# Two units of an inverse transform moved between stages of the next half, and the loads and products for that half made earlier, in a long-convolution and MLP kernel

## The reference, cut to what matters

```python
h_filt = (np.maximum(pos_emb @ w1, 0.0) @ w2) * window        # 12480 x 128
u = x * v
Uf = np.fft.rfft(u, n=2 * S, axis=1)                          # S = 12480
Hf = np.fft.rfft(h_filt, n=2 * S, axis=0)
y = np.fft.irfft(Uf * Hf[None, :, :], n=2 * S, axis=1)[:, :S, :]
x = x * y                                                      # then 12480 tokens of 128
x = np.maximum(x @ moe_w_in, 0.0) ** 2 @ moe_w_out             # 128 -> 2048 -> 128
h = x @ moe2_w_in
out = h * (1 / (1 + np.exp(-1.702 * h))) @ moe2_w_out
```

## Time and profile before

| what | value |
|---|---|
| timed runs | 1421.34 us median; 1411.77, 1421.34, 1422.18 |
| profiled execution | 1423.75 us, of which the span 1421.9 us |
| TensorE busy | 1411.5 us (99%), mean granted clock 0.993 |
| first half: stages 1, 2, 3, 4 begin at | 20.3, 65.6, 136.9, 165.7 us |
| second half: stages 1, 2, 3, 4 begin at | 202.65, 229.1, 276.85, 305.6 us |
| first MLP matmul | 323.5 us |

### The profile page before, as it was taken

The page is one execution under the profiler, slowest core; times in us unless marked ns, Lnnn a source line. Parts: engine busy times, 40 slices in busy tenths (PEclk is TensorE's granted clock), DMA queues, the critical chain, the costliest instruction groups (busy, mean ns, idle before and its releaser), DMA issues.

```text
span 1421.9 us, 22644 instructions
## 1 busy us (share of the span) xinstructions
PE 1411.5 (99%) x8370; PEld 1398.4 (98%) x8370; DVE 851.5 (60%) x1092; ACT 1000.6 (70%) x1422; POOL 190.2 (13%) x157
## 2 busy tenths in 40 slices
PE   9999999999999999999999999999999999999999
PEld 9999999999999999999999999999999999999998
DVE  6745416745666666666666666666666666666664
ACT  7654325555877777777777777777777777777776
POOL 5545533551000000000000000000000000000000
PEclk9999979999999999999999999999999999999999
DMA  8254352642000000000000000000000000000000
GB/s 250 67 160 125 81 143 70 187 139 76 0 19 19 18 18 18 18 18 18 18 18 18 18 18 18 18 18 18 18 18 18 18 18 18 18 18 18 6 7 12
DMA packets 32646, 63.75 MB, mean 45 GB/s; under 512 B 3964, under 2 KB 24876, under 8 KB 32348
## 3 DMA queue, kind: packets, MB, share of 16 engines
q1 hardware_dynamic: 32064, 62.76, 15.4%
q10 hardware_dynamic: 540, 0.42, 0.1%
HBM read 50.38 MB, written 6.39 MB: 40 GB/s over the span
## 4 chain that ended last, share of the span: by engine, by line
PE 96%; DMA 2%; ACT 1%; DVE 1%; issue 0%; POOL 0%; POOLq 0%; ACTq 0%
PE ps L1106 25%; PE ps L1108 25%; PE ps L1107 25%; PE ps L792 5%; PE ps L802 4%; PE ps L423 3%; PE ps L849 3%; PE ps L855 3%; PE ps L827 1%; DMA f_ring<-in_inv 1%; ACT big L596 1%; DMA f_ring<-in_fwd 0%; POOL big L380 0%; PE ps L773 0%; PE ps L808 0%
## 5 line engine op out<-in xcount | busy, mean ns | idle before, releaser
L1094 DVE TENSOR_TENSOR act_lo<-act_f,act_hi 128x832 fp32r<-128x832 f32 x480 | 487.9, 1027 | 120.9 <-ACT act_hi L1050 112.7
L1106 PE MATMUL ps<-act_hi,w_hi 128*128 128x416 f32 x960 | 338.4, 353 | 0.7 <-DVE act_lo L1094 0.7
L1106 PE MATMUL ps<-in_hi,w_hi 128*128 128x416 f32 x960 | 336.6, 351 | 0.0
L1107 PE MATMUL ps<-act_lo,w_hi 128*128 128x416 f32 x960 | 336.2, 350 | 0.0
L1108 PE MATMUL ps<-act_hi,w_lo 128*128 128x416 f32 x960 | 336.0, 350 | 0.0
L1108 PE MATMUL ps<-in_hi,w_lo 128*128 128x416 f32 x960 | 335.6, 350 | 0.0
L1107 PE MATMUL ps<-in_lo,w_hi 128*128 128x416 f32 x960 | 335.0, 349 | 0.0
L1092 DVE CAST act_hi<-act_f 128x832 fp32r<-128x832 f32 x240 | 142.6, 594 | 291.8 <-ACT act_f L1045 291.8
L1040 ACT ACTIVATE relu<-ps 128x832 f32<-128x832 f32 x240 | 208.1, 867 | 130.7 <-PE ps L1108 126.6
L1047 ACT ACTIVATE act_f<-ps 128x832 f32<-128x832 f32 x240 | 207.4, 864 | 102.1 <-PE ps L1108 102.1
L1045 ACT ACTIVATE act_f<-relu 128x832 f32<-128x832 f32 x240 | 216.1, 900 | 21.8
(11 more groups left out here) (74 smaller groups left out, 1089.5 us busy)
## 6 DMA issues: line engine op xcount, KB each, us to landing
f_ring<-in_fwd SPq DMA_DIRECT2D x52, 240.0 KB, 2.7
big<-in_inv SPq DMA_DIRECT2D x26, 338.0 KB
big<-in_x_by_channel SPq DMA_DIRECT2D x16, 390.0 KB
big<-in_v_by_channel SPq DMA_DIRECT2D x16, 390.0 KB
x_tile<-in_x_by_tile SPq DMA_DIRECT2D x30, 208.0 KB, 2.7
xy_tile<-big SPq DMA_DIRECT2D x60, 104.0 KB, 2.5
out<-yT SPq DMA_DIRECT2D x30, 208.0 KB, 1.9
big<-in_pos_by_pair SPq DMA_DIRECT2D x15, 208.0 KB, 5.3
```

What stands on the lines that cost most here:

```text
L1094: nc.vector.tensor_tensor(lo[:, :, :], f[:, :, :], hi[:, :, :].bitcast(F32), ALU.subtract)\
L1106: nc.tensor.matmul(to, w_hi[w][:, cols], hi, start=first, stop=False)
L1107: nc.tensor.matmul(to, w_hi[w][:, cols], lo, start=False, stop=False)
```

## The change

- Units 13 and 14 (`KEPT`) of the first half's stage 4 are done in the second half: unit 13 in PSUM slot 1 between stages 1 and 2, unit 14 in slot 2 between stages 2 and 3. Their rows of `Y`, their tables and the last table stay in SBUF till then; for that `h_spec`, `by_re` and `by_im` have other places in the second half.
- The tables have 12 places in the first half; tables 12, 13 and 14 go to the places of 0, 2 and 3 (`T4_AGAIN`). Tables 2, 3 and the last lie over the staging of x and v.
- x and v of pieces 0 to 4 are loaded at two different steps of stage 2; pieces 5 to 7 in stage 3, piece 7 in piece 6's place. GpSimd makes pieces 0 to 3 between its additions of stage 2, and doesn't wait for the stage's end before piece 4.
- The raw weights 0 and 1 are loaded after the second half's stage 2, between tables.
- The last group of stage 2 is split into 8 and 56 channels (before: 32 and 32), and TensorE waits for the second part at step 2 of stage 3 (before: 8).
- The last group of stage 3 is split: VectorE does the first 12 rows of `Y` first and signals `y_first`; stage 4 waits for that and for three of the four slots.
- Spare products: none before the second half's stages 2 and 3, three of one each at the other stage ends.

```diff
 XV_AT = (...,
-         [XV_TOP - (PIECES_AHEAD - i) * XV for i in (*range(PIECES_AHEAD), 4, 3, 4)])
+         [XV_TOP - (PIECES_AHEAD - i) * XV for i in (*range(PIECES_AHEAD), 3, 4, 4)])
+BY_AT = SPEC_AT + 2 * 3 * FG * HC, P1_END
+KEPT_T4_AT = P1_END + 2 * 2 * 2 * FG * HC
+H_SPEC_AT = SPEC_AT, IM_AT
+KEPT = JG - 2, JG - 1
+S4_UNITS = JG - len(KEPT), JG - LATE
+KEPT_SLOT = 1, 2
...
-    t4_places = [[(ring_rows, n * TB * TAB) for n in range(2)]
+    t4_places = [[(ring_rows, n * TB * TAB) for n in range(2)] + [(big, KEPT_T4_AT + n * TB * TAB) for n in range(2)]
                  + [(big, X_AT[0] + X_SIZE + n * TB * TAB) for n in range(8)],
...
+    T4_AGAIN = {T4S[0]: 0, T4S[0] + 1: 2, T4S[0] + 2: 3}
...
-    PARTS = [slice(0, HC // 2), slice(HC // 2, HC)]
+    PARTS = [slice(0, PC), slice(PC, HC)]
+    FIRST_ROWS = (RING - 1) * TB
...
-    def y_made(eng, h):
+    def y_begun(eng, h):
 
-        for q in range(RING):
+        for q in range(RING - 1):
             eng.wait_ge(free[q], used["s3 end", h][q])
+        eng.wait_ge(y_first, h + 1)
...
         for k in range(RING, NG):
             load_f(0, k)
-            if k % RING == RING - 1:
-                load_u(1, k // RING - 1)
+            if k % 2 and k // RING <= PIECES_AHEAD:
+                load_u(1, k // RING - 1, (k % RING // 2,))
 
         p_made(sp, 0)
         stage_done(sp, "s2", 0)
         for g in range(2):
             load_t4(sp, 0, g)
+        for i, consumed in ((5, 3), (6, 4), (7, 6)):
+            sp.wait_ge(u_folded, PIECES + consumed + 1)
+            load_u(1, i)
+        sp.dma_start(w2bd, out_net[:, 2 + D:]).then_inc(w2_in, 16)
+        sp.wait_ge(u_folded, 2 * PIECES)
+        for g in range(2, 4):
+            load_t4(sp, 0, g)
         sp.dma_start(t4_last[0], inv4[:, JG * TB * TAB:]).then_inc(t4_last_in, 16)
-        sp.dma_start(w2bd, out_net[:, 2 + D:]).then_inc(w2_in, 16)
 
         stage_done(sp, "s3", 0)
-        for g in range(2, T4S[0]):
+        for g in range(4, T4S[0]):
             load_t4(sp, 0, g)
-        sp.wait_ge(u_folded, PIECES + 4 + 1)
-        load_u(1, 5)
         load_t4_behind(0, range(T4S[0], JG))
-        sp.wait_ge(u_folded, PIECES + 3 + 1)
-        load_u(1, 6)
-        sp.wait_ge(u_folded, PIECES + 5 + 1)
-        load_u(1, 7)
 
         stage_done(sp, "s4", 0)
         for k in range(NG):
             load_f(1, k)
-        for m in range(2):
-            load_w(m)
-
         p_made(sp, 1)
+        sp.wait_ge(p_rest, 2)
+        load_w(0)
         stage_done(sp, "s2", 1)
-        for g in range(T4S[1]):
+        for g in range(2):
+            load_t4(sp, 1, g)
+        sp.wait_ge(full[KEPT_SLOT[1]], used["kept", 1] + 1)
+        load_w(1)
+        for g in range(2, T4S[1]):
             load_t4(sp, 1, g)
...
                 combine_p(nc.gpsimd.tensor_tensor, k, h, k % 2)
+                i, step = k // RING - 2, k % RING
+                if h == 0 and 0 <= i < PIECES_AHEAD - 1:
+                    if step == 0:
+                        multiply(1, i)
+                    elif step < 3:
+                        fold(1, i, step - 1)
             if h == 0:
 
-                p_made(pool, 0)
-                stage_done(pool, "s2", 0)
-                for i in range(PIECES):
+                for i in range(PIECES_AHEAD - 1, PIECES):
                     make_u(1, i)
...
+        def keep_kept(unit):
+
+            q = KEPT_SLOT[unit]
+            act.wait_ge(full[q], used["kept", unit] + 1)
+            keep_xy(nc.scalar.copy, 0, KEPT[unit], q).then_inc(free[q], 1)
...
             step1_odd(k, h, *act_copies(k, h)).then_inc(last_odd, 1)
+            if h == 1:
+                keep_kept(0)
...
             copy_last_h()
+            if h == 1:
+                keep_kept(1)
             act.wait_ge(p_rest, h + 1)
...
                 dve.wait_ge(im_copied, h * N3 + k + 1)
+                if k == N3 - 1:
+                    rows = slice(0, FIRST_ROWS)
+                    nc.vector.tensor_tensor(low[:, :, rows], re2[:, :, rows], im2[:, :, rows], ALU.subtract)
+                    nc.vector.tensor_tensor(high[:, :, rows], re2[:, :, rows], im2[:, :, rows], ALU.add).then_inc(y_first, 1)
+                    low, high, re2, im2 = (rows[:, :, FIRST_ROWS:] for rows in (low, high, re2, im2))
...
+        def step4_kept(unit):
+
+            q = KEPT_SLOT[unit]
+            pe.wait_ge(free[q], used["kept", unit])
+            step4(pe, 0, KEPT[unit], q, full[q])
...
+            else:
+                step4_kept(0)
             for s in range(RING):
-                if h == 0 and s % 2 == 0:
+                if h == 0 and s % 2 == 0 or h == 1 and s == KEPT_SLOT[0]:
                     continue
                 pe.wait_ge(free[s], used["s1 end", h][s])
-                if h == 1 and s < RING - 1:
-                    spare_products(s, 1)
...
-            for k, spare in ((NG - 4, 2), (NG - 3, 1), (NG - 2, 2)):
-                q, n = product_slot(k, 1)
-                if h == 0:
-                    q, n = hidden_slot(k)
-                    before, m = product_slot(k - 1, 0)
-                    pe.wait_ge(free[before], m + 1)
+            if h == 1:
+                step4_kept(1)
+            for k in (NG - 4, NG - 3, NG - 2) if h == 0 else ():
+                q, n = hidden_slot(k)
+                before, m = product_slot(k - 1, 0)
+                pe.wait_ge(free[before], m + 1)
                 pe.wait_ge(free[q], n + 1)
-                spare_products(q, spare)
+                spare_products(q, 1)
             p_made(pe, h)
 
             for k in range(N3):
-                if k == N3 // 2:
+                if k == PC // 4:
                     pe.wait_ge(p_rest, h + 1)
                 step3(k, h)
 
-            for k, spare in ((N3 - 4, 1), (N3 - 3, 2), (N3 - 2, 2)):
+            for k, spare in ((N3 - 4, 1), (N3 - 3, 1), (N3 - 2, 1)):
...
-            y_made(pe, h)
-            for g in range(JG - h * LATE):
+            y_begun(pe, h)
+            for g in range(S4_UNITS[h]):
```

More of the change, by code:

```diff
@@ L273, in convolution, with t4_slot @@
     T4S = [len(slots) for slots in t4]
-    T4_USES = [len(range(n, JG, T4S[0])) for n in range(T4S[0])]
-    t4_last = [ring_rows[:, 2 * TB * TAB:2 * TB * TAB + TAB], big[0:A, T4_AT[1] + 5 * TB * TAB:W_LO2_AT]]
+    T4_AGAIN = {T4S[0]: 0, T4S[0] + 1: 2, T4S[0] + 2: 3}
+    T4_USES = [1 + (n in T4_AGAIN.values()) for n in range(T4S[0])]
+    t4_last = [big[0:A, at:at + TAB] for at in (KEPT_T4_AT + 2 * TB * TAB, T4_AT[1] + 5 * TB * TAB)]
+    def t4_slot(h, g):
+        if h:
+            return g % T4S[1], T4_USES[g % T4S[1]] + g // T4S[1] + 1
+        return (T4_AGAIN[g], 2) if g in T4_AGAIN else (g, 1)
     def x_and_v(h, i):
@@ L312, in convolution @@
     last_copied, part_negated = sem("last_copied"), sems("part_negated", 2)
-    part_made, p_rest = sem("part_made"), sem("p_rest")
+    part_made, p_rest, y_first = sem("part_made"), sem("p_rest"), sem("y_first")
     p_done = sems("p_done", 2)
@@ L318, in convolution @@
     for h in range(2):
-        for name, groups in (("s1", N1[h]), ("s2", (2 - h) * NG), ("s3", N3), ("s4", JG - h * LATE)):
+        for name, groups in (("s1", N1[h]), ("s2", (2 - h) * NG), ("s3", N3), ("s4", S4_UNITS[h])):
             used[name, h] = list(n)
@@ L322, in convolution @@
             used[name + " end", h] = list(n)
+            if h == 1 and name in ("s1", "s2"):
+                unit = ("s1", "s2").index(name)
+                used["kept", unit] = n[KEPT_SLOT[unit]]
+                n[KEPT_SLOT[unit]] += 1
     F_USES = [len(range(s, NG, RING)) for s in range(RING)]
@@ L373, in product_slot @@
         return q, used["s2", h][q] + (k // RING if h else k // 2)
-    PARTS = [slice(0, HC // 2), slice(HC // 2, HC)]
+    PARTS = [slice(0, PC), slice(PC, HC)]
+    FIRST_ROWS = (RING - 1) * TB
     def combine_p(tensor_tensor, k, h, half):
         to = P[h][:, :, :, k * FG:(k + 1) * FG].rearrange("p c r f -> p r c f")
-        tensor_tensor(to, by_re[:, half], by_im[:, half], ALU.add).then_inc(p_done[half], 1)
+        tensor_tensor(to, by_re[h][:, half], by_im[h][:, half], ALU.add).then_inc(p_done[half], 1)
     def after(eng, sem, n):
@@ L412, in step4 @@
     def step4(pe, h, g, q, done):
[L414 to L415 removed]
+        n, loads = t4_slot(h, g)
+        pe.wait_ge(t4_in[n], 16 * loads)
         blocks = [(0, i, t4[h][n][:, i]) for i in range(TB)]
@@ L462, in load_pe, with load_u @@
                 .then_inc(ld_pe[n], 16)
-        def load_u(h, i):
+        def load_u(h, i, both=(0, 1)):
             c = h * HC + i * PC
-            for to, rows in zip(x_and_v(h, i), (x_ch, v_ch)):
-                sp.dma_start(to, rows[:, c:c + PC, :]).then_inc(ld_u[i], 16)
+            for n in both:
+                sp.dma_start(x_and_v(h, i)[n], (x_ch, v_ch)[n][:, c:c + PC, :]).then_inc(ld_u[i], 16)
         def load_f(h, k):
@@ L545, in _, with multiply, fold, make_u @@
     def _(pool):
-        def make_u(h, i):
+        def multiply(h, i):
```

(22 more changed lines are left out.)

18 lines of the change are left out of this document (9 added, 9 removed).

## The result

The changed kernel takes 1429.9 us (six runs, 1428.6 to 1430.8). Before takes 1413.4 (six runs, 1411.4 to 1422.2, with the three known ones among them). The ratio is 1.0104, with a 95% interval of 1.0077 to 1.0131: slower by 1.0%, where I forecast 1405. Two things are in that number. The changed kernel loses 23 us in one place (its profile shows the place; its six runs lie within 2.2 us of each other), and before doesn't usually lose the 10 us of clock that I took out of it: over all series 17 of its 64 runs lie at 1421 or more, the others between 1411 and 1415.

The account below looks back on a forecast made before the run. TensorE, busy 99% of the span, was taken to bound the kernel. From the profiled execution, 1423.75-12.0-0.3-3.65-1.6+0.5+0.15=1406.8, a usual run 2 under: 1405 us; range 1401 to 1419.

Parts of the forecast that it names:

- The tables' queue: SyncE's loads for the first half's stage four: table 2 lands 0.5 us before its need; 0.5 us of later waits.
- the rival: First half's stage four: table 2 late, TensorE idles 1.5 us at unit 2, clock falls; 1424 us, chance 0.12.
- 12.0 us on one transfer: First half's stage four in before: a late table costs 2.0 us idle plus the clock's fall; all 12.0 go.
- The price of the fall: Lower clock in before: 7.5 us in stage four's last 84 records, 2.5 us in the second half's stage one.
- The units: Units 13 and 14 moved from the first half's stage four into the second half's gaps: net -3.65 us.
- First rows: End of stage three: first rows done apart start stage four 0.8 us earlier in both halves, -1.6 us.
- U made in stage two: First half: GpSimd's pieces 0 to 3 fit between its combines of stage two, cost zero.
- The 0.3 us for the forward table: Loading x and v at different steps may remove a 0.4 us table wait; 0.3 us gain taken.
- Weights 0 and 1 later: Second half: loading them between tables from about 278.5 costs zero, with ScalarE up to 2 us late.
- First channels: Start of stage three: 8 and 56 channels gain nothing, cost zero up to 0.5; 0.15 us added.
- Spare products: Stage-end gaps: fewer of them cost no time, since other engines end those gaps.
- rival b: Start of stage three: VectorE's first add loses to GpSimd's product, TensorE idles some 3 us; 1450 us, chance 0.06.

Follow-up runs that it names:

- experiment 1: Changed kernel with table places swapped: tables 2 to 9 where P was, 10, 11 and the last over the staging of x and v; 1406.4 us.
- experiment 2: Changed kernel with pieces 5 and 6 of x and v issued ahead of tables 0 and 1 in the first half's stage three; 1406.7 us.
- experiment 5: The kernel before, unchanged, run for a second profile; 1412.2 us (one run).
- experiment 4: The kernel before with piece 5 of x and v issued behind tables 10 to 13 instead of ahead of table 10; 1412.6 us, ratio 0.9972.
- experiment 12: Kernel of 8 with the first rows apart undone and five spare products (1, 2, 2) before the first half's stage four; 1406.7 us.
- 8: Kernel of experiment 1 with the first half's last two stage-four units in order 12, 11 and table 12 issued ahead of 11; 1405.6 us.
- experiment 10: Kernel of 8 with the first channels apart undone (32 and 32, second part wanted at step 8); 1405.7 us.
- experiment 9: Kernel of 8 with the first rows apart undone, three spare products kept before stage four; 1406.6 us in one run, 1427.8 to 1427.9 in three.
- experiment 6: Changed kernel with three spare products in front of unit 2 of the first half's stage four; six runs 1408.0 to 1410.0, four 1427.9 to 1430.9 us.
- experiment 3: Changed kernel with eight spare products in front of unit 2 of the first half's stage four, table 2 still late; 1409.2 us.

## Why the prediction was wrong

**The step that failed** is in "The tables' queue": "Table 2 lands at 168.0", with a margin of 0.5 us. Stage three began at 135.95 instead of 136.9, so in this trace's times I had piece 5 at 144.4, the last fold at 163.9, table 2 at 167.1 and the need at 167.6. Measured: piece 5 at 146.15 (+1.7), piece 7 5.9 us after its issue (+0.6), table 2 3.7 us after its own (+0.5). That is 2.8 us late against 0.5 of margin. GpSimd's 4.7 us per piece, the need and the order of events were right. The term that was too small is the landing time of a piece. It came from one median landing of a 240 KB load plus bytes over a mean rate, and three such prices stand one behind the other in a chain in which each piece waits for the one before.

Three things show what was missing. First, experiments 1 and 2 show that the chain decides: with table 2 outside it, or with piece 5 issued first, the wait is gone. Second, a piece with nothing ahead of it takes 5.9 to 6.4 us (piece 7 in the profile after, pieces 5 and 7 in experiment 2), not 5.3. Third, piece 5 didn't have the queue to itself behind the two tables: some 0.6 MB of piece 6 went over before it had landed, and my sum stopped at piece 5's own bytes. How much of the 1.7 us this last part makes is open; no run holds piece 6 back. The prediction had a row that would have warned it: it worked out 1.86 us per table for before, where other loads stood behind too, and used that for the tables from number 2 on, but the faster 209 GB/s (1.66 us per table) for the pieces. At 1.86 us per 338 KB piece 5 would have landed 9.4 us after the issue, piece 7 after 5.7, and table 2 would have been late by 0.8 us.

**The second error is of weighing.** The prediction had the rival and its mechanism, at 1424 us and a chance of 0.12, and I took the margin as if it were safe. I gave the chance that GpSimd is 1 us late too little, and the range ended at 1419. Its size was off by 6 us: the wait was 2.4 and not 1.5, the fall cost 18.0 in the units and not 15.6, 2.9 and not 2.5 in stage one, and the kernel without it takes 1406.4 and not 1405. The price of the units was low because the factor 1.79 was taken from 84 records of before of which the first ran at full clock: the means over windows of 1 us (1.00 for 186 to 187, 0.64 for 187 to 188) put the fall near 187.3, 1.5 us behind the wait's end. In the changed kernel the fall came at once, and the factor is 37.84/19.85=1.91.

**Before as the base.** I read the fall in the profiled run of before as its usual state (12.0 us on one transfer). It is in 17 of 64 runs; the profile of experiment 5 has 1.0 us of waiting and no fall. The price of the fall held: there the 84 records take 9.60 us and stage one 22.54, which is 9.9 us less than in the first profile, where I had 10.0. Taking the table wait out of before gained nothing that its interval settles (experiment 4). One of the three times that I had, 1411.77, was a run without it; I named it, and still took the difference from the slower two. Against the usual 1413 a flawless change was worth 7 to 8 us, 0.5%, and never over 1%.

**What held.** With table 2 in time the kernel takes 1406.4 (experiment 1), 1405.6 with the 0.7 us wait for slot 0 gone; my sum was 1405. That it comes so near is in part luck, since it left out that wait and had 0.5 us of table waits that none of these runs has. From before's usual profile (1412.2 with 1.0 us of table wait) the terms give 1412.2-1.0-3.0-1.6=1406.6 for experiment 1. I had missed the wait for slot 0: with 13 units the last one sits in slot 0, in which the next stage begins. The units: 3.0 once that wait is taken off, measured 2.9. The gap before the second half's stage three is filled exactly, and TensorE goes from unit 14 into stage three without a pause (its timeline):

```profile
281.39 2.38 PE L442 MATMUL ps<-big 104*128 104x104 f32 x20
283.61 1.60 PE L859 MATMUL ps<-t,big 120*104 120x120 f32 x14
```

First rows: 1.6 forecast, 1.1 measured in time (experiment 12 against 8). The traces show the 0.8 in each half: stage four begins 1.54 us behind the last matmul of stage three with the rows apart and 2.32 with them together. The rest of the difference lies in front: in the profile of 12 stage three began at 135.46, in that of 8 at 135.89. U made in stage two: no wait of TensorE in that stage. The 0.3 us for the forward table isn't shown: that wait is not in the list of after, but it isn't in that of before's second profile (experiment 5) either, where stage three began at 136.22 instead of 136.89. Weights 0 and 1 later: no wait. First channels: I counted nothing, and 0.3 us is in the traces, because in before the 0.49 us of "issue" behind the combine were really VectorE's add; the time doesn't resolve it.

**Spare products: right for this kernel, with half the reason.** I priced fewer of them at nothing because other engines end those gaps, and named the clock only for the gap in front of stage three. That gap was idle for 0.8 us (1.1 in experiment 10) without a fall. Experiments 9 and 12 show what they do in front of stage four: with the rows together, three instead of five cost 21 us in three of four runs.

**The add and the product** (rival b): the first add waited for the combine, which ends at 135.77, and ran ahead of the product (timeline of both engines):

```profile
135.40 0.45 DVE L796 TENSOR_TENSOR big<-big 120x64 f32<-120x64 f32 x1
...
135.79 2.22 POOL L573 TENSOR_TENSOR big<-big 104x960 f32<-104x960 f32 x1
...
136.95 1.54 DVE L796 TENSOR_TENSOR big<-big 120x448 f32<-120x448 f32 x1
```

64 elements took 0.45 us, twice the 0.23 of their products, and the second add (448 elements) took 1.54 under the product. The Trainium skill (SBUF — State Buffer, "Who interferes with whom") says that a VectorE instruction with two SBUF inputs contends with a GpSimd one that reads SBUF; both of these lengths agree.

## What to carry to other kernels

When a load is moved behind a chain of other work (land, compute, free a place, load again), price each landing from a row for the same bytes under the same traffic, with the bytes of every load that will be issued before it lands, and count the margin against the sum of the errors, not against zero. If a wait in a stage can bring TensorE's clock down, its cost isn't its length (here 2.4 us against 23), so give the tables that are needed first the places that come free first. And look at all the timed runs of the base before attributing a state that one profile shows.

## What the runs showed of the hardware

- Idle pieces of TensorE just before or in the first half's stage four, and the clock behind them: 0.8 us, no fall in five runs (experiment 12); 1.0, none in the one run of experiment 5; 1.4, a fall in three of four runs (experiment 9); 1.6, in four of ten (experiment 6); 2.0, a fall in the first profile of before; 2.4, in all six of the changed kernel. Each length is that of the one profiled run; those of the others aren't known. Experiment 9's profile has a fall behind 1.41 us in the first half and none behind 1.38 us in the second. That the length of the idle piece alone doesn't decide it is likely and not shown; what else does, these runs leave open.
- The clock of the same kernel before fell in 2 of 6, 5 of 18, 10 of 23, 0 of 9 and 0 of 8 runs of the five series. So a count of falls from one series says little of another.
- By the means over windows of 1 us (an estimate) the clock fell as soon as work began again behind the 2.4 us, and 1.4 to 2.0 us later behind the 1.4, 1.6 and 2.0 us (experiments 9, 6, before).
- Once at 1.2 GHz, TensorE stayed there through 41.5 us of uninterrupted stage four (experiment 9, clock 0.50 from 166.0 to 207.5) and came back only in stage one. In the changed kernel the clock is 0.50 from 170.1 to 208.0 and 0.88 on the mean of the following stage.
- A load issued some 4 us behind another on the same queue (piece 6 at 140.74, piece 5 at 136.72) moved some 0.6 MB before that other one had landed (profile after, 135.90 to 146.10: 2.08 MB, of which 1.49 belong to what was issued first).
- Eight unread matmuls (2.46 us) in the place of an idle piece saved 20.7 us (experiment 3 against the changed kernel).
